# An expert layer's block loop on TensorE: the first product placed ahead of the wait for the plan, and one plan number read a block in place of two

## The reference, cut to what matters

```python
def _moe2_ref(x, w_skip, w_gate, w1, w2):     # N, D, E, F = 3072, 384, 8, 1024
    do_compute = x @ w_skip > 0
    xc = x[do_compute]
    logits = xc @ w_gate
    e_idx = np.argmax(logits, axis=1)
    ...                                        # gate_w: softmax weight of the chosen expert
    for e in range(E):
        mask = e_idx == e
        h = np.maximum(xc[mask] @ w1[e], 0.0)
        y[mask] = gate_w[mask, None] * (h @ w2[e])
    out[do_compute] = xc + y
```

## Time and profile before

| | us |
|---|---|
| timed runs | 728.21, 728.44, 720.26 (median 728.21) |
| profiled execution, its own time | 721.34 |
| its span, first to last instruction | 719.5 |
| TensorE matmuls busy | 686.2 (95%) |
| TensorE weight loads busy | 645.4 (90%) |
| VectorE busy | 413.5 (57%) |
| ScalarE busy | 306.9 (43%) |
| mean granted TensorE clock | 0.986 |

### The profile page before, as it was taken

How to read it: one execution, slowest core, us unless ns; L and a number is a source line. 1 busy time by engine, 2 the same in 40 slices (tenths; PEclk the granted TensorE clock), 3 DMA queues, 4 the chain that set the end, 5 groups by cost and what they waited for, 6 DMA issues and landing times.

```text
span 719.5 us, 14041 instructions
## 1 busy us (share of the span) xinstructions
PE 686.2 (95%) x4361; PEld 645.4 (90%) x4362; DVE 413.5 (57%) x862; ACT 306.9 (43%) x665; POOL 84.8 (12%) x110
## 2 busy tenths in 40 slices
PE   8989999999999999999999999999997999999993
PEld 7989999999999999999999999999993778888883
DVE  8875756645656565555657555534557562655751
ACT  4535434434334443343444335333442452735550
POOL 6430000100010010001000100100101113222311
PEclk9999999999999999999999999999999899999997
DMA  8826624220422421142222222006014881462400
GB/s 248 256 87 198 198 67 133 67 64 15 129 61 66 124 75 27 45 130 65 67 68 82 59 61 86 12 18 235 12 53 160 303 310 51 149 248 84 165 20 8
DMA packets 38585, 77.43 MB, mean 108 GB/s; under 512 B 8472, under 2 KB 26806, under 8 KB 38528
## 3 DMA queue, kind: packets, MB, share of 16 engines
q1 hardware_dynamic: 33632, 62.37, 28.0%
q10 hardware_dynamic: 2432, 9.76, 3.7%
q0 software_dynamic: 2464, 4.58, 2.1%
HBM read 61.09 MB, written 12.41 MB: 102 GB/s over the span
## 4 chain that ended last, share of the span: by engine, by line
PE 87%; DVE 6%; issue 3%; ACT 2%; ACTq 0%; DVEq 0%; POOL 0%; POOLq 0%
PE bank L703 29%; PE bank L721 27%; PE bank L852 8%; PE bank L808 7%; PE bank L585 4%; PE bank L641 3%; PE bank L636 3%; PE bank L654 2%; PE bank L836 2%; PE bank L679 1%; PE bank L623 1%; DVE h_sb L1232 1%; PE bank L800 1%; ACT h_sb L947 0%; ACT w_hi L976 0%
## 5 line engine op out<-in xcount | busy, mean ns | idle before, releaser
L1232 DVE TENSOR_TENSOR h_sb<-h_sb,bank 128x384 f32<-128x384 f32 x128 | 70.9, 554 | 168.9 <-ACT h_sb L947 163.7
L947 ACT ACTIVATE h_sb<-bank 128x384 f32<-128x384 f32 x128 | 62.9, 491 | 245.1 <-PE bank L703 235.0
L703 PE MATMUL bank<-x_hi,win_hi 128*128 128x384 f32 x384 | 134.4, 350 | 2.4 <-DVE win_lo L1254 1.9
L721 PE MATMUL bank<-wout_hi,g_hi 128*128 128x394 f32 x384 | 131.5, 342 | 0.0
L721 PE MATMUL bank<-wout_hi,g_lo 128*128 128x394 f32 x384 | 131.4, 342 | 0.0
L721 PE MATMUL bank<-wout_lo,g_hi 128*128 128x394 f32 x384 | 131.3, 342 | 0.0
L703 PE MATMUL bank<-x_hi,win_lo 128*128 128x384 f32 x384 | 129.4, 337 | 0.0
L703 PE MATMUL bank<-x_lo,win_hi 128*128 128x384 f32 x384 | 129.2, 336 | 0.0
L1239 DVE TENSOR_TENSOR g_lo<-h_sb,g_hi 128x384 fp32r<-128x384 f32 x128 | 71.3, 557 | 33.4 <-ACT g_hi L954 32.2
L954 ACT ACTIVATE g_hi<-h_sb 128x384 fp32r<-128x384 f32 x128 | 66.6, 520 | 44.6 <-DVE h_sb L1232 41.3
L703 PEld LDWEIGHTS bank<-x_hi,win_hi 128*128 128x128 f32 x384 | 72.1, 188 | 8.9 <-issue 6.5
(11 more groups left out here) (207 smaller groups left out, 972.4 us busy)
## 6 DMA issues: line engine op xcount, KB each, us to landing
raw<-in_experts SPq DMA_DIRECT2D x32, 768.0 KB, 6.3
rkt<-in_rk_t SPq DMA_DIRECT2D x46, 192.0 KB
rkn<-in_rk_nat SPq DMA_DIRECT2D x21, 384.0 KB
v<-in_v_nat SPq DMA_DIRECT2D x24, 192.0 KB, 2.9
z_rows<-z_sb SPq DMA_DIRECT2D x24, 192.0 KB, 2.7
out<-z_sb SPq DMA_DIRECT2D x24, 192.0 KB, 2.9
stage<-in_win ACTq DMA_DIRECT2D x4, 768.0 KB, 4.4
stage<-in_wout_t ACTq DMA_DIRECT2D x4, 768.0 KB, 6.2
```

The costliest lines, as they stand in the source:

```text
L703: mm = pe.matmul(h_ps[t % 2][:, 0:GT], a[:, kk, cols], b[G % 2][:, kk, :], start=n == 0, stop=n == 3 * KT - 1)
L721: mm = pe.matmul(z_ps[i][:, 0:ZW], a[t % 3][:, tok], b[:, f, :], start=f == 0 and j == 0, stop=f == FT - 1 and j == 2)
L947: act.activation(h_sb[t % 2][:], h_ps[t % 2][:, 0:GT], ACT.Copy, scale=SLOPE).then_inc(s_h_scaled, 1)
L1232: dve.tensor_tensor(h_sb[t % 2][:], h_sb[t % 2][:], h_ps[t % 2][:, 0:GT], ALU.max).then_inc(s_leaky, 1)
```

## The change

The wait for the plan and the read of the number of blocks go behind block 0's first product. In the loop, the two reads of PARITY are gone: the parity is worked out as the expert's number modulo 2. The read of cur goes from the head of the block to the place behind the first product's issue, and odd with it. Nothing else differs; the other engines' programs are the same.

```diff
-            pe.wait_ge(s_plan_done, 1)
-            blocks = pe.value_load(plan[0:1, TOTAL:TOTAL + 1], min_val=E, max_val=BLOCKS)
             pe.wait_ge(rows_in[0], 16)
             turn_rows(0)
             pe.wait_ge(s_zt_lo, 1)
             first_product(0, 0, 0)
+            pe.wait_ge(s_plan_done, 1)
+            blocks = pe.value_load(plan[0:1, TOTAL:TOTAL + 1], min_val=E, max_val=BLOCKS)
             pe.wait_ge(rows_in[1], 16)
             turn_rows(1)
...
                             nxt = pe.value_load(plan[0:1, bass.ds(EXPERT + j + 1, 1)], min_val=0,
                                                 max_val=E - 1)
-                            nxt_odd = pe.value_load(plan[0:1, bass.ds(PARITY + j + 1, 1)], min_val=0,
-                                                    max_val=1)
-                            cur = pe.value_load(plan[0:1, bass.ds(EXPERT + j, 1)], min_val=0, max_val=E - 1)
-                            odd = pe.value_load(plan[0:1, bass.ds(PARITY + j, 1)], min_val=0, max_val=1)
+                            nxt_odd = nxt % 2
 
                             pe.wait_ge(s_relu_done, j + 1)
                             for f in range(EFT):
...
                                 first_product((u + 1) % 2, nxt_odd * EW, PIECES * nxt)
+
+                            cur = pe.value_load(plan[0:1, bass.ds(EXPERT + j, 1)], min_val=0, max_val=E - 1)
+                            odd = cur % 2
 
                             with pe.If(j < blocks - 2):
```

## The result

The changed kernel is faster by 1.2%: over 20 runs of each the medians are 716.20 and 724.79 us, and the ratio is 0.9878 with a 95% interval of 0.9851 to 0.9904. That is 8.8 us (7.0 to 10.8) where 6.8 were forecast. The ratio is of the runs within 1.5% of each kernel's fastest, so it is not exactly that of the medians, which lie 8.6 us apart. The first three runs of the kernel before, 728.21, 728.44 and 720.26, from which the forecast started, have a median 3.4 us above that of the 20; so 721.4 was forecast and 716.2 came out, inside the range of 712 to 727.

The account below looks back on a forecast made before the run. TensorE bounds the expert stage, stalled by four plan reads at each block's head. The loop's 6.1 us plus the opening's 0.7 make 6.8; 728.21 - 6.8 = 721.4 us, range 712 to 727.

Parts of the forecast that it names:

- Stalls by reads at the head: Before hidden-value transposes, blocks 1 to 13: four plan reads cost 3.0 us; removing three moves readiness 2.15 us, closing every stall.
- branches nor the hand-over: Rival at the block heads: loop branches and hand-over, not reads, make the stalls; only the opening gains, 727.5 us; chance 0.05.
- What is late next: In the block loop, VectorE's weight splitting limits some blocks, so 6.1 of 8.05 us of closed stalls count.
- The moved read at no cost: Behind line 808's product: reading cur and parity takes 0.85 us of sequencer, covered by 18 queued products (4.12 us); cost 0.
- The opening: Block 0's first product starts 0.97 us earlier, limited by ScalarE's own plan read; 0.7 us gained at its end.
- The clock: Low stretch in the opening expected to stay; last block's 24 products taken as no change, bounds +1.6 and -2.6 us.
- The rival of a better clock: Clock high in both the opening and the last block: 11.1 us gained, 717.1 us; chance 0.08.
- That all 8 us count: Rival in the block loop: VectorE's chains move along too, so 8.05 + 0.7 = 8.8 us, 719.4; chance 0.10.
- the modulo: Rival at lines 852 and 808: parity redone at each address as several operations, slowing the kernel to 749 us; chance 0.04.
- as cheap as 0.2: Rival at the block heads: reads priced lower, 0.6 us a block, so stalls shrink without closing, 723.6 us; chance 0.07.
- The 200 ns: Rule for a register load at the block heads: three reads 0.6 us a block, total gain 4.6 us instead of 6.8.

Follow-up runs that it names:

- loop alone: Changed kernel with the wait and read of blocks put back ahead of block 0's turned rows; ratio 0.9917 against the kernel before, median 717.47 us.
- both at the head: Changed kernel with cur read at the block's head right after nxt, none behind the first product; ratio 0.9872 against the kernel before.
- opening alone: Kernel before with only the plan wait and read of blocks moved behind block 0's first product; ratio 1.0005.
- Filling the last gap: Two unused products before the last block's 24 products; ratios 0.9965 on the kernel before, 0.9889 on the changed kernel.

## Why the prediction was right

**Stalls by reads at the head: right.** All 13 closed with 1.2 to 2.2 us to spare (0.8 in the worst forecast); four reads, and neither branches nor the hand-over, made them (loop alone; both at the head).

**What is late next: right, its sum better than its parts.** 6.1 us of 8.05 were to count, 6.06 did. Where the stalls were said to be lost they were: the stretch from block 4's transposes to block 5's, for one, is shorter by 0.17 us, one step, and line 808 in block 5 waits 0.28 for w1_lo. By parts it went otherwise in several places. Behind block 2 the rows landed late (0.4 us at line 800), and nothing was gained where 0.16 were forecast; blocks 10 and 11 together gave 0.57 rather than 0.84, since line 852 of block 10 waited longer for eht_lo. Blocks 4 and 5 gave 0.98 rather than 0.78, blocks 8 and 9 1.59 rather than 1.38, blocks 12 and 13 1.23 rather than 1.12. The transposes themselves, unstalled, start over 0.76 us rather than 0.82, which the sum had not. That these offset each other to 0.04 us is luck.

**The moved read at no cost: right, for a reason put too simply.** "2.2 us ahead" was read in block 0, between line 852's addresses and its products. From the start of the read to TensorE's next step it is 3.3 to 4.1 us in most blocks and 1.6 in blocks 5, 9 and 12, as two reads at that place showed. One read fits, five did not.

**The opening: right in mechanism.** The first product started 1.14 us earlier, 0.98 when counted from VectorE's last plan step (0.97 forecast), held by ScalarE's read: with ScalarE's and VectorE's steps ahead of their reads it moved by 0.9 more. In the profiled pair the low stretch kept half of it: 0.5 gained at its end, 0.3 from the plan step (0.7 forecast). In the other profiles of this opening 1.5 to 3.2 us are gained at that place, as the low stretch is shorter or absent; it was as long as before in one profile of seven. In time the opening alone is not measurable.

**The clock: the term of the sum that was mis-sized.** The text put "no change" for the last block. In the profiled pair it was 1.35 us; over all runs the changed kernels' clock was higher by 0.004, worth 2.5 us, and the gain was 8.8 rather than 6.8. The rival of a better clock (717.1) names the effect, in the opening and in the last block. Which of the two it was, or neither, stays open. The profiles tie the last block's low stretch to no edit: it is absent in the opening alone, which keeps all 13 stalls, and present in four kernels that have none. Filling the last gap gave no clear answer. In the opening the changed order had shorter stretches in most profiles, but the 12 runs of the opening alone have no better mean clock. Much of the clock's spread also lies far ahead, in the first 100 us.

**The other rivals.** That all 8 us count is refuted by the waits that took their place; the modulo costs no time on TensorE, since line 852 still takes 4.1 to 4.2 us a block, and 0.05 us of sequencer at the first address of line 852 and of line 808 in a block, not once per address; the stall of 1.38 us in block 8 was closed whole, so the read is not as cheap as 0.2. The 200 ns that the Trainium skill gives for a register load ("Runtime: NRT & Kernel Launch", section "Instruction fetch mechanics") would have closed an estimated 0.6 us a block; the runs don't bear it out here. The page speaks there of loads that the runtime adds around a kernel; a read of the tile plan takes 0.30 us for its load alone.

## What to carry to other kernels

An engine's sequencer has its own critical path: where a block begins with several reads of a plan, compare their time (0.65 to 0.75 us each here) with what is still queued on the engine at that point, and spread them over places that have cover. The cover is not one number; it is shortest just behind an instruction that had itself to wait (1.6 us here, against 3.3 to 4.1 elsewhere). When such a stall is closed, read which engine the next wait names, because the same cheap edit there (2.9 us more at equal clock) may be worth half as much again. And a profile is one execution: before a low stretch of the clock is put down to an edit, look whether it comes and goes in the profiles of kernels that have the same code at that place.

## What the runs showed of the hardware that was not expected

- The spread of the runs within one kernel, 720 to 737 us over the 57 of the kernel before, is nearly all clock: about 1 us of scatter is left about the line. Much of what differs lies in the first 100 us, which no edit here touches: the granted clock from 0 to 110 us was 0.98 in the profiles of the kernel before and of the changed one, 0.92 in those with the opening or the loop alone.
- Repeated reads at one address were started every 0.65 us (four from 621.0 to 623.5), where reads at different places took 0.75.
- `% 2` added no register operation of its own: the counts at lines 808 and 852 stayed, and no instruction stands on the line of the modulo. It went into an operation that was there. The first register operation of line 852 in a block takes 104 ns in the changed kernel, 51 before (14 of 112), that of line 808 99 to 113 ns, 46 before (13 of 78); with both parities read it is 46 to 51 ns at both lines again.
- Eight transposes whose weight loads run ahead start over 0.76 us, stalled ones over 0.82.
